# Two dense layers behind an FFT filter on one core: input loads on one queue, eight warm products, another order at the seam and in the last pair

## The chip, the cores and the metric

The kernel runs on one core of a Trainium2 chip. The metric is the device time of one execution in microseconds, taken as the median of several runs. The engines are named as the profile names them: PE (TensorE, matrix products), PEld (its weight loads), DVE (VectorE), ACT (ScalarE), POOL (GpSimd) and SP (SyncE, which here only issues DMAs).

## The reference

```python
X = np.fft.rfft(x, axis=1)                  # x: 2 x 3008 x 256
Y = X * (filt_r + 1j * filt_i)[None, :, :]
x = np.fft.irfft(Y, n=3008, axis=1).reshape(6016, 256)
h = x @ moe_w_in                            # 256 -> 2048
x = np.maximum(0.01 * h, h) @ moe_w_out     # 2048 -> 256
h = x @ moe2_w_in
r = np.maximum(h, 0.0)
out = (r * r) @ moe2_w_out                  # 6016 x 256
```

## The kernel before

**Stage one, the Fourier filter.** 3008 is cut into 64 x 47. The input `X` (128 rows, two batches, 24 steps `m` of 256 channels) comes in 16 pieces, eight for each batch, of 2, 2, 2, 2, 4, 4, 4 and 4 steps (`XG`); a piece of two steps has 256 KB, one of four 512 KB. SP issues 14 of them (L216); pieces 1 and 3 of batch 0 are issued by ACT (`X_BY_ACT`, L506), whose queue also carries the three small matrices `DM`: the first, for the products over n1, ahead of them (L503) and the other two behind them (L507). `over_n1(c, half)` (L872 to L881) is a chunk of four products of 128 columns, one for each step `m`; in single precision each is two instructions in the trace. For the first eight chunks half 0 and half 1 alternate; half 0 waits for a piece of `X` where a step begins one. Ahead of all that PE runs ten products on a cleared tile `WARM` (L869), which DVE clears (L744) and which nothing reads. Then follow, for 32 units, a transposition (`turn`, L895), the products with the tables `TB` (`spectrum`, L906), the filter on DVE and POOL, and the way back (`inverse`, L916), with a trip through memory (`zu`), and at last 24 chunks `sequence(c)` (L934) that give the 6016 tokens in `YT`. ACT and DVE copy these chunks out of PSUM (`y_copy`, lists `Y_ACT` and `Y_DVE`).

**Stages two and three, the dense layers.** The tokens are handled in six pairs of blocks for each layer (five of 2 x 512 tokens and one of 2 x 448), each pair in `KU` = 8 steps over the 2048 hidden values, so there are `SLOTS` = 96 steps `s`. Each 2 x 2 block product is done with seven products instead of eight, by sums of blocks, and each operand is split into a rounded part and a rest (`XH` and `YL`/`XL`, `WIH` and `WIL`, `GH` and `GL`), so that each product is three passes on PE (L973 to L975 upward; L965 to L967 downward). A step has the groups a, b, c and d upward and four down groups, of kinds `UA`, `UB`, `UC`, `UD`, six products each. `UA` and `UC` add to token block 0 (PSUM banks 4 and 5), `UB` and `UD` to block 1 (banks 6 and 7). `down(n)` runs `LAG` = 6 groups behind. The order on every engine is written out by hand, with semaphores for the waits.

**The seam.** Stage two needs pair 0 of the tokens in its forms: sums `x0_t` on DVE, roundings `x_round0(1..6)` on ACT (L561 to L567), rests `x_split0(1..6)` on DVE (L762 to L768). Group a of step 0 waits for rests 1 and 2, group b for 3 and 4, group d for 6. The last four chunks of `sequence` are put between these groups. In each step ACT copies two half-finished products out of PSUM: `snap1` (L621) and `snap2` (L628, into `SN`). Group c, which goes on adding to the same bank, waits for `snap2` (semaphore `s2u_sb`).

```python
            for n in range(4 * SLOTS - LAG, 4 * SLOTS):
                down(n)
```

**The end.** With these two lines PE ends: the last six down groups in the order of their numbers. The result of the last pair leaves in three stores, all issued by SP: block 0 whole, after a copy on ACT (`evacuate(2 * NP - 1, 0)`, L657, both banks in one instruction); row half 0 of block 1, after a copy on DVE (L863), which waits for the first half of the last group; and row half 1 of block 1, after a copy on ACT (L706). SP then waits until all stores have landed.

Of the kernel before, what the change touches and what calls it, by code (L numbers as in the profile page):

```python
# [17 lines left out]
NP = len(PAIR_W)  # L18
KU = FCH // 2
SLOTS = 2 * NP * KU  # L20
XG = (2, 2, 2, 2, 4, 4, 4, 4)
# [7 lines left out]
def fft_mlp_kernel(nc, x, filt, dft, tab, w1i, w1o, w2i, w2o, out):  # L29
# [60 lines left out]
    with ExitStack() as ctx:  # L90
# [75 lines left out]
        Y_ACT = tuple(c for c in range(2 * CH) if c not in Y_DVE)  # L166
        FILL = 2 * CH - 4
        X_START = [sum(XG[:g]) for g in range(len(XG))]
        X_BY_ACT = ((0, 1), (0, 3))
        CHUNKS = 4 * KU  # L170
        W2_IN = (0, 5, 6, 7)
        LATE = 4
# [38 lines left out]
        def _(sp):  # L211
            def load_x(b):
                for g, n in enumerate(XG):
                    m = X_START[g]
                    if (b, g) not in X_BY_ACT:
                        sp.dma_start(X[:, b, m:m + n, :], x[:, b, m:m + n, :]).then_inc(x_in[b][g], 16)  # L216

            def load_filter(f):
                if f >= FSLOTS:
# [3 lines left out]
            def load_table(u):  # L223
                if u in (0, PAIRS - 2):
                    for half in range(2):
                        sp.wait_ge(n1_ps[half], CH // 2 if u == 0 else CH // 2 + 1)
                sp.dma_start(TB[:, u, :, :], tab[:, u, :, :]).then_inc(tb_in[u], 16)
# [19 lines left out]

            load_x(0)
            load_x(1)
            load_table(0)  # L250
            load_table(1)
            load_filter(0)
# [73 lines left out]

            c, w = pair_cols(2 * NP - 1)
            sp.wait_ge(evac[0], 2 * NP)
            sp.dma_start(out[:, :, c:c + w], YT[:, :, c:c + w]).then_inc(out_done, 16)
            sp.wait_ge(last_evac, 1)  # L330
            sp.dma_start(out[:, 0, c + w:c + 2 * w], YT[:, 0, c + w:c + 2 * w]).then_inc(out_done, 16)
            sp.wait_ge(evac[1], 2 * NP)
            sp.dma_start(out[:, 1, c + w:c + 2 * w], YT[:, 1, c + w:c + 2 * w]).then_inc(out_done, 16)
            sp.wait_ge(out_done, 16 * (NP + 2))

        @block.gpsimd
        def _(pool):

            pool.wait_ge(n1_ps[1], CH - LATE + 2)
            nc.gpsimd.memset(XF[32:IM, :, :, :], 0.0).then_inc(xf_pad, 1)  # L340

# [159 lines left out]
        @block.scalar  # L501
        def _(act):
            act.dma_start(DM[:, 0, :], dft[:, 0, :]).then_inc(dft_in, 16)  # L503
            for b, g in X_BY_ACT:
                m, n = X_START[g], XG[g]
                act.dma_start(X[:, b, m:m + n, :], x[:, b, m:m + n, :]).then_inc(x_in[b][g], 16)  # L506
            act.dma_start(DM[:, 1:3, :], dft[:, 1:3, :]).then_inc(dft_rest, 16)  # L507

            for c in range(CH):
                act.wait_ge(n1_ps[0], c + 1)  # L510
# [24 lines left out]
            def wo_round(k):  # L535
                act.wait_ge(wo_raw[k], 16)
                nc.scalar.activation(WOH[:, k, :], WOF[:, wo_slot(k), :], ACT.Copy).then_inc(wo_hi, 1)
# [64 lines left out]
            for c in Y_ACT:  # L602
                if DRAIN <= c < FILL:
                    y_copy(c)
                if c in (4, 6):
                    wi_round(WI_UNITS + (c - 4) // 2)
                if c in (8, 10):
                    wo_round((c - 8) // 2)
                if c == 15:
                    x_round0(1)  # L610
                    x_round0(2)
                if c == 16:
                    x_round0(3)
# [9 lines left out]
            def snap2(s):  # L623

                act.wait_ge(p6_ps, s + 1)
                if s >= 1:
                    act.wait_ge(h_sb[UC], s)
                nc.scalar.activation(SN[:, 0:width(s)], PS[:, XB[s % 2], 0:width(s)], ACT.Copy).then_inc(s2u_sb, 1)  # L628
# [30 lines left out]
            for s in range(SLOTS + 1):  # L659
# [14 lines left out]
                if s == 0:  # L674
                    x_round0(5)
                    x_round0(6)
                    snap2(0)
                if s < SLOTS:
                    g_round(s, UA)
                if k == 1 and p >= 1:  # L680
                    evacuate(p - 1, 1)
                if 1 <= s < SLOTS:
                    snap2(s)
                if s >= 1:
                    g_round(s - 1, UD)
# [15 lines left out]
                    w2_round(s - KU)  # L701

            c, w = pair_cols(2 * NP - 1)
            evacuate(2 * NP - 1, 0)
            act.wait_ge(down_ps, 4 * SLOTS)
            nc.scalar.activation(YT[:, 1, c + w:c + 2 * w], PS[:, 7, 0:w], ACT.Copy).then_inc(evac[1], 1)  # L706

        @block.vector
        def _(dve):
# [28 lines left out]
            def y_copy(c):  # L738

                y, ps = y_cols(c)  # L740
                dve.wait_ge(y_ps, c + 1)
                nc.vector.tensor_copy(y, ps).then_inc(y_done(c)[0], 1)  # L742

            nc.vector.memset(WARM[:, :], 0.0).then_inc(warm_sb, 1)  # L744
            for c in range(CH - 2):
                n1_copy(c)
            filtered(0)
# [35 lines left out]
            nc.vector.tensor_tensor(b12, b22, b12, ALU.subtract).then_inc(x0_t, 1)  # L783
            y_copy(17)
            x_split0(3)
            y_copy(19)
            dve.wait_ge(x0_t, 4)
            x_split0(4)

            def whole_a(s):  # L790

# [67 lines left out]
                    y_copy(23)  # L859

            c, w = pair_cols(2 * NP - 1)
            dve.wait_ge(last_ps, 1)
            nc.vector.tensor_copy(YT[:, 0, c + w:c + 2 * w], PS[:, 6, 0:w]).then_inc(last_evac, 1)  # L863

        @block.tensor
        def _(pe):
            pe.wait_ge(warm_sb, 1)
            for _ in range(10):
                nc.tensor.matmul(PS[:, 0, 0:128], WARM[:, :], WARM[:, :], start=True, stop=True)  # L869
            pe.wait_ge(dft_in, 16)  # L870

# [199 lines left out]
                    sequence(FILL + 3)  # L1071
                down(4 * s - LAG + 3)
            group_d(SLOTS - 1)
            for n in range(4 * SLOTS - LAG, 4 * SLOTS):
                down(n)


def dft_tables():
# [116 lines left out]
```

## Time and profile before

| | us |
|---|---|
| median of 3 runs (lowest, highest) | 1089.81 (1089.57, 1090.07) |
| the profiled execution: its own time | 1089.14 |
| its span | 1087.4 |
| PE busy in it | 1081.5 (99%) |
| DVE, ACT, POOL busy | 771.8, 567.5, 294.9 |

The span runs from the first to the last instruction; 1.7 us of the profiled execution lie outside it. A busy PE is not a PE at its peak: its products overlap, and one that starts late because a clock or an operand was late still counts as busy. So what counts here is when successive products start, and rows of the timeline show that.

### The profile page before, as it was taken

To read this page: it belongs to the slowest core of one execution; us is meant where nothing else is said; L and a number is where in the kernel's file an instruction comes from. 1 tells how busy PE (TensorE), PEld (TensorE's weight loads), DVE (VectorE), ACT (ScalarE), POOL (GpSimd) and SP (SyncE) were. 2 spreads that over 40 slices of the span, in tenths; PEclk is the share of its full clock that TensorE was granted. 3 is DMA by queue.
4 is the path that set the end of the run, shared out by engine and by line. 5 is a ranking of instruction groups with operands and counts; after the bars stand their busy time and mean duration, and the time that the engine had idled before them with its cause. 6 is when DMAs were issued, how large, how long until landed. Compare 5 with 4: busy or idle time off the path is not lost.

```text
span 1087.4 us, 14076 instructions
## 1 busy us (share of the span) xinstructions
PE 1081.5 (99%) x5108; PEld 914.0 (84%) x5108; DVE 771.8 (71%) x1184; ACT 567.5 (52%) x983; POOL 294.9 (27%) x285
## 2 busy tenths in 40 slices
PE   9999999999999999999999999999999999999998
PEld 9888888888888888888899888888888888888997
DVE  2996889777677677676666776776766766766665
ACT  3556655565565565565454554554554554554543
POOL 0789344224234234224220220220220220120000
PEclk9999999999999999999999999999999999999999
DMA  9778400012112212212144200000000000000000
GB/s 319 222 217 274 151 1 1 22 44 59 44 44 54 49 44 54 48 44 55 54 159 158 73 1 1 39 1 1 39 1 1 39 1 1 39 1 1 39 1 34
DMA packets 70053, 66.09 MB, mean 61 GB/s; under 512 B 40800, under 2 KB 55648, under 8 KB 69984
## 3 DMA queue, kind: packets, MB, share of 16 engines
q1 hardware_dynamic: 69408, 64.47, 19.2%
q8 instruction: 41, 0.67, 0.2%
q10 hardware_dynamic: 576, 0.72, 0.2%
q14 instruction: 28, 0.23, 0.1%
HBM read 41.19 MB, written 23.99 MB: 60 GB/s over the span
## 4 chain that ended last, share of the span: by engine, by line
PE 98%; DMA 1%; DVE 1%; ACT 0%; issue 0%; ACTq 0%; DVEq 0%
PE PS L967 16%; PE PS L966 16%; PE PS L965 16%; PE PS L973 14%; PE PS L975 14%; PE PS L974 14%; PE PS L906 3%; PE PS L916 3%; PE PS L879 2%; PE PS L934 1%; PE PS L895 1%; DMA X<-in_x 1%; DVE YL L762 0%; DVE YT L742 0%; DVE XT L780 0%
## 5 line engine op out<-in xcount | busy, mean ns | idle before, releaser
L650 ACT ACTIVATE GH<-GF 128x512 fp32r<-128x512 f32 (+1 forms) x384 | 238.8, 622 | 225.3 <-DVE GF L822 116.3
L828 DVE TENSOR_TENSOR GL<-GF,GH 128x512 fp32r<-128x512 f32 (+1 forms) x384 | 258.6, 680 | 105.2 <-ACT GH L650 99.3
L967 PE MATMUL PS<-GH,WOL 128*128 128x512 f32 (+1 forms) x768 | 295.8, 385 | 0.0
L965 PE MATMUL PS<-GH,WOH 128*128 128x512 f32 (+1 forms) x768 | 295.8, 385 | 0.0
L966 PE MATMUL PS<-GL,WOH 128*128 128x512 f32 (+1 forms) x768 | 295.8, 385 | 0.0
L973 PE MATMUL PS<-XH,WIH 128*128 128x512 f32 (+1 forms) x672 | 259.8, 387 | 0.1
L975 PE MATMUL PS<-XH,WIL 128*128 128x512 f32 (+1 forms) x672 | 258.8, 385 | 0.0
L796 DVE TENSOR_TENSOR GF<-PS,GF 128x512 f32<-128x512 f32 (+1 forms) x96 | 65.3, 680 | 163.8 <-ACT GF L621 163.7
L966 PEld LDWEIGHTS PS<-GL,WOH 128*128 128x128 f32 x768 | 144.2, 188 | 26.9
L965 PEld LDWEIGHTS PS<-GH,WOH 128*128 128x128 f32 x768 | 144.2, 188 | 26.9
L967 PEld LDWEIGHTS PS<-GH,WOL 128*128 128x128 f32 x768 | 144.2, 188 | 26.8
L974 PE MATMUL PS<-YL,WIH 128*128 128x512 f32 (+1 forms) x384 | 147.8, 385 | 0.0
L973 PEld LDWEIGHTS PS<-XH,WIH 128*128 128x128 f32 x672 | 126.2, 188 | 25.7 <-ACT SN L628 1.4
L975 PEld LDWEIGHTS PS<-XH,WIL 128*128 128x128 f32 x672 | 126.1, 188 | 23.5
L621 ACT ACTIVATE GF<-PS 128x512 f32<-128x512 f32 (+1 forms) x96 | 56.5, 588 | 167.0 <-PE PS L967 166.0
L820 DVE SCALAR_TENSOR_TENSOR GF<-GF 128x512 f32<-128x512 f32 (+1 forms) x192 | 142.2, 780 | 1.7
L822 DVE SCALAR_TENSOR_TENSOR GF<-GF 128x512 f32<-128x512 f32 (+1 forms) x192 | 121.6, 673 | 1.7
L974 PE MATMUL PS<-XL,WIH 128*128 128x512 f32 (+1 forms) x288 | 111.0, 385 | 0.0
L421 POOL TENSOR_TENSOR YL<-YT,XH 128x1024 fp32r<-128x1024 f32 (+1 forms) x22 | 52.6, 2390 | 137.9 <-DVE GL L828 137.9
L644 ACT ACTIVATE GF<-PS 128x512 f32<-128x512 f32 (+1 forms) x96 | 56.8, 591 | 57.5 <-PE PS L975 57.5
L974 PEld LDWEIGHTS PS<-YL,WIH 128*128 128x128 f32 x384 | 72.1, 188 | 13.3
L804 DVE TENSOR_TENSOR GF<-PS,GF 128x512 f32<-128x512 f32 (+1 forms) x96 | 64.4, 671 | 0.0
(74 smaller groups left out, 959.1 us busy)
## 6 DMA issues: line engine op xcount, KB each, us to landing
zu<-U SPq DMA_DIRECT2D x32, 192.0 KB, 2.8
V<-zu SPq DMA_DIRECT2D x12, 512.0 KB, 5.4
FL<-in_filt SPq DMA_DIRECT2D x16, 336.0 KB, 4.9
out_y<-YT SPq DMA_DIRECT2D x5, 1024.0 KB, 4.3
X<-in_x SPq DMA_DIRECT2D x8, 512.0 KB, 9.7
wi<-PWH SPq DMA_DIRECT2D x16, 224.0 KB, 2.5
wi<-PWL SPq DMA_DIRECT2D x16, 224.0 KB, 3.1
WIH<-wi SPq DMA_DIRECT2D x8, 448.0 KB, 3.5
```

Of the source, the lines that this page charges most:

```text
L650: nc.scalar.activation(GH[:, g, 0:width(s)], GF[:, g, 0:width(s)], ACT.Copy).then_inc(g_hi[kind], 1)
L796: nc.vector.tensor_tensor(h, PS[:, YB, 0:w], h, ALU.add).then_inc(h_sb[UA], 1)
L804: nc.vector.tensor_tensor(h, PS[:, XB[s % 2], 0:w], h, ALU.add).then_inc(h_sb[UB], 1)
L820: nc.vector.scalar_tensor_tensor(h, h, 0.01, h, ALU.mult, ALU.max).then_inc(g_sb[kind], 1)
L822: nc.vector.scalar_tensor_tensor(h, h, 0.0, h, ALU.max, ALU.mult).then_inc(g_sb[kind], 1)
L828: nc.vector.tensor_tensor(GL[:, g, 0:w], GF[:, g, 0:w], GH[:, g, 0:w].bitcast(f32), ALU.subtract).then_inc(g_lo[kind], 1)
L965: nc.tensor.matmul(acc, wh, xh, start=first, stop=False)
L966: nc.tensor.matmul(acc, wh, xl, start=False, stop=False)
L967: return nc.tensor.matmul(acc, wl, xh, start=False, stop=last)
L973: nc.tensor.matmul(acc, wh, xh, start=first, stop=False, skip_group_check=not first)
L974: nc.tensor.matmul(acc, wh, lo, start=False, stop=False, skip_group_check=not first)
L975: return nc.tensor.matmul(acc, wl, xh, start=False, stop=True, skip_group_check=not first)
```

## The change

- SP issues all 16 pieces of `X` in order, and behind them the second part of `DM`. ACT issues only the first matrix.
- `WARM` is cleared by POOL and no longer by DVE, and PE runs eight products on it and not ten.
- At the seam ACT does `x_round0(1)` ahead of the copy of chunk 15 and not behind it, and in step 1 `snap2(1)` ahead of the rounding `g_round(1, UA)`. DVE does `x_split0(4)` ahead of the copy of chunk 19.
- In the last step the down groups run as UA, UC, UB, UD. Block 0 of the last pair is copied by two engines (ACT bank 4, DVE bank 5) as soon as UC is done and is stored then. The store of row half 1 of block 1 is issued by ACT, on ACT's own queue, right behind ACT's copy.

```diff
--- before.py
+++ after.py
@@ -166,7 +166,6 @@
         Y_ACT = tuple(c for c in range(2 * CH) if c not in Y_DVE)
         FILL = 2 * CH - 4
         X_START = [sum(XG[:g]) for g in range(len(XG))]
-        X_BY_ACT = ((0, 1), (0, 3))
         CHUNKS = 4 * KU
         W2_IN = (0, 5, 6, 7)
         LATE = 4
@@ -212,8 +211,7 @@
             def load_x(b):
                 for g, n in enumerate(XG):
                     m = X_START[g]
-                    if (b, g) not in X_BY_ACT:
-                        sp.dma_start(X[:, b, m:m + n, :], x[:, b, m:m + n, :]).then_inc(x_in[b][g], 16)
+                    sp.dma_start(X[:, b, m:m + n, :], x[:, b, m:m + n, :]).then_inc(x_in[b][g], 16)
 
             def load_filter(f):
                 if f >= FSLOTS:
@@ -247,6 +245,7 @@
 
             load_x(0)
             load_x(1)
+            sp.dma_start(DM[:, 1:3, :], dft[:, 1:3, :]).then_inc(dft_rest, 16)
             load_table(0)
             load_table(1)
             load_filter(0)
@@ -326,16 +325,16 @@
 
             c, w = pair_cols(2 * NP - 1)
             sp.wait_ge(evac[0], 2 * NP)
+            sp.wait_ge(last_evac, 1)
             sp.dma_start(out[:, :, c:c + w], YT[:, :, c:c + w]).then_inc(out_done, 16)
-            sp.wait_ge(last_evac, 1)
+            sp.wait_ge(last_evac, 2)
             sp.dma_start(out[:, 0, c + w:c + 2 * w], YT[:, 0, c + w:c + 2 * w]).then_inc(out_done, 16)
-            sp.wait_ge(evac[1], 2 * NP)
-            sp.dma_start(out[:, 1, c + w:c + 2 * w], YT[:, 1, c + w:c + 2 * w]).then_inc(out_done, 16)
             sp.wait_ge(out_done, 16 * (NP + 2))
 
         @block.gpsimd
         def _(pool):
 
+            nc.gpsimd.memset(WARM[:, :], 0.0).then_inc(warm_sb, 1)
             pool.wait_ge(n1_ps[1], CH - LATE + 2)
             nc.gpsimd.memset(XF[32:IM, :, :, :], 0.0).then_inc(xf_pad, 1)
 
@@ -501,10 +500,6 @@
         @block.scalar
         def _(act):
             act.dma_start(DM[:, 0, :], dft[:, 0, :]).then_inc(dft_in, 16)
-            for b, g in X_BY_ACT:
-                m, n = X_START[g], XG[g]
-                act.dma_start(X[:, b, m:m + n, :], x[:, b, m:m + n, :]).then_inc(x_in[b][g], 16)
-            act.dma_start(DM[:, 1:3, :], dft[:, 1:3, :]).then_inc(dft_rest, 16)
 
             for c in range(CH):
                 act.wait_ge(n1_ps[0], c + 1)
@@ -606,8 +601,9 @@
                     wi_round(WI_UNITS + (c - 4) // 2)
                 if c in (8, 10):
                     wo_round((c - 8) // 2)
+                if c == 14:
+                    x_round0(1)
                 if c == 15:
-                    x_round0(1)
                     x_round0(2)
                 if c == 16:
                     x_round0(3)
@@ -674,12 +670,13 @@
                 if s == 0:
                     x_round0(5)
                     x_round0(6)
-                    snap2(0)
+                if s < 2:
+                    snap2(s)
                 if s < SLOTS:
                     g_round(s, UA)
                 if k == 1 and p >= 1:
                     evacuate(p - 1, 1)
-                if 1 <= s < SLOTS:
+                if 2 <= s < SLOTS:
                     snap2(s)
                 if s >= 1:
                     g_round(s - 1, UD)
@@ -701,9 +698,12 @@
                     w2_round(s - KU)
 
             c, w = pair_cols(2 * NP - 1)
-            evacuate(2 * NP - 1, 0)
+            act.wait_ge(down_ps, 4 * SLOTS - 2)
+            nc.scalar.activation(YT[:, 0, c:c + w], PS[:, 4, 0:w], ACT.Copy).then_inc(evac[0], 1)
             act.wait_ge(down_ps, 4 * SLOTS)
             nc.scalar.activation(YT[:, 1, c + w:c + 2 * w], PS[:, 7, 0:w], ACT.Copy).then_inc(evac[1], 1)
+            act.wait_ge(evac[1], 2 * NP)
+            act.dma_start(out[:, 1, c + w:c + 2 * w], YT[:, 1, c + w:c + 2 * w]).then_inc(out_done, 16)
 
         @block.vector
         def _(dve):
@@ -741,7 +741,6 @@
                 dve.wait_ge(y_ps, c + 1)
                 nc.vector.tensor_copy(y, ps).then_inc(y_done(c)[0], 1)
 
-            nc.vector.memset(WARM[:, :], 0.0).then_inc(warm_sb, 1)
             for c in range(CH - 2):
                 n1_copy(c)
             filtered(0)
@@ -783,9 +782,9 @@
             nc.vector.tensor_tensor(b12, b22, b12, ALU.subtract).then_inc(x0_t, 1)
             y_copy(17)
             x_split0(3)
-            y_copy(19)
             dve.wait_ge(x0_t, 4)
             x_split0(4)
+            y_copy(19)
 
             def whole_a(s):
 
@@ -859,13 +858,15 @@
                     y_copy(23)
 
             c, w = pair_cols(2 * NP - 1)
+            dve.wait_ge(down_ps, 4 * SLOTS - 2)
+            nc.vector.tensor_copy(YT[:, 1, c:c + w], PS[:, 5, 0:w]).then_inc(last_evac, 1)
             dve.wait_ge(last_ps, 1)
             nc.vector.tensor_copy(YT[:, 0, c + w:c + 2 * w], PS[:, 6, 0:w]).then_inc(last_evac, 1)
 
         @block.tensor
         def _(pe):
             pe.wait_ge(warm_sb, 1)
-            for _ in range(10):
+            for _ in range(8):
                 nc.tensor.matmul(PS[:, 0, 0:128], WARM[:, :], WARM[:, :], start=True, stop=True)
             pe.wait_ge(dft_in, 16)
 
@@ -1071,8 +1072,10 @@
                     sequence(FILL + 3)
                 down(4 * s - LAG + 3)
             group_d(SLOTS - 1)
-            for n in range(4 * SLOTS - LAG, 4 * SLOTS):
+            for n in range(4 * SLOTS - LAG, 4 * SLOTS - 4):
                 down(n)
+            for kind in (UA, UC, UB, UD):
+                down(unit(SLOTS - 1, kind))
 
 
 def dft_tables():
```

The input loads on SP, before and then changed. `X<-in_x 128x512` is a piece of two steps, `128x1024` one of four, `in_dft` the small matrices:

```order
0 L210 UNCONDITIONAL_BRANCH
1 L216 DMA X<-in_x 128x512 x2
2 L216 DMA X<-in_x 128x1024 x4
3 L216 DMA X<-in_x 128x512 x4
4 L216 DMA X<-in_x 128x1024 x4
5 L227 DMA TB<-in_tab 112x416 x2
```

```order
0 L209 UNCONDITIONAL_BRANCH
1 L214 DMA X<-in_x 128x512 x4
2 L214 DMA X<-in_x 128x1024 x4
3 L214 DMA X<-in_x 128x512 x4
4 L214 DMA X<-in_x 128x1024 x4
5 L248 DMA DM<-in_dft 128x256
```

Two small pieces came to SP's queue ahead of the four large ones of batch 0, and the rest of `DM` stands between `X` and the tables.

DVE at the seam, before and then changed. `YL<-YT,XH_69` are rests (`x_split0` 2 and 4), `XL_71` is rest 3, `COPY YT<-PS` copies chunks 17 and 19, `GF<-PS,GF` is the first sum of step 0:

```order
107 L783 TENSOR_TENSOR YT<-YT 128x512
108 L742 COPY YT<-PS 128x512 [waits y_ps]
109 L765 TENSOR_TENSOR XL_71<-XT_73,XH_69 128x1024 [waits x0_hi]
110 L742 COPY YT<-PS 128x512 [waits y_ps]
111 L762 TENSOR_TENSOR YL<-YT,XH_69 128x512 [waits x0_hi,x0_t]
112 L796 TENSOR_TENSOR GF<-PS,GF 128x512 [waits s1_sb,p2_ps]
```

```order
106 L782 TENSOR_TENSOR YT<-YT 128x512
107 L742 COPY YT<-PS 128x512 [waits y_ps]
108 L764 TENSOR_TENSOR XL_71<-XT_73,XH_69 128x1024 [waits x0_hi]
109 L761 TENSOR_TENSOR YL<-YT,XH_69 128x512 [waits x0_hi,x0_t]
110 L742 COPY YT<-PS 128x512 [waits y_ps]
111 L795 TENSOR_TENSOR GF<-PS,GF 128x512 [waits s1_sb,p2_ps]
```

The rest and the copy of chunk 19 changed places; nothing else moved there.

ACT in steps 0 and 1, before and then changed. `SN<-PS` is `snap2(1)`, `GH<-GF` are roundings (the letter behind `g_sb` is the kind), `GF<-PS` with `p3_ps` is the copy for kind UD:

```order
104 L650 ACTIVATE GH<-GF 128x512 [waits g_sb_b]
105 L644 ACTIVATE GF<-PS 128x512 [waits p3_ps]
106 L650 ACTIVATE GH<-GF 128x512 [waits g_sb_a]
107 L628 ACTIVATE SN<-PS 128x512 [waits h_sb_c,p6_ps]
108 L650 ACTIVATE GH<-GF 128x512 [waits g_sb_d]
```

```order
103 L646 ACTIVATE GH<-GF 128x512 [waits g_sb_b]
104 L640 ACTIVATE GF<-PS 128x512 [waits p3_ps]
105 L624 ACTIVATE SN<-PS 128x512 [waits h_sb_c,p6_ps]
106 L646 ACTIVATE GH<-GF 128x512 [waits g_sb_a]
107 L646 ACTIVATE GH<-GF 128x512 [waits g_sb_d]
```

`snap2(1)` moved ahead of one rounding.

## Rows read from the trace of the kernel before

**Rows 1.** The page: the chain that ended last, by engine.
```profile
PE 98%; DMA 1%; DVE 1%; ACT 0%; issue 0%; ACTq 0%; DVEq 0%
```

**Rows 2.** Timeline 0 to 30 us: start, duration, engine, line, tiles, count, idle before.
```profile
0.83 0.17 DVE L744 MEMSET WARM<- 128x128 f32 x1 [0.83 <-PEq L1186]
1.05 4.64 PE L869 MATMUL PS<-WARM 128*128 128x128 f32 x20 [1.05 <-DVE WARM L744]
5.48 2.84 PE L879 MATMUL PS<-DM,X 128*128 128x128 f32 x20
8.77 16.85 PE L879 MATMUL PS<-DM,X 128*128 128x128 f32 x148 [0.44 <-DMA X<-in_x]
27.01 1.37 POOL L340 MEMSET XF<- 32x1536 f32 x1 [26.57 <-PE PS L879]
```

**Rows 3.** Windows: stretch, length, busy and starts by engine, PEclk, DMA share, GB/s.
```profile
5.00:6.00 1.00, 1.00 (x7) 1.00 (x6) 0.00 (x0) 0.00 (x0) 0.00 (x0) 1.00 0.99 346
7.00:8.00 1.00, 1.00 (x11) 1.00 (x11) 0.08 (x1) 0.60 (x1) 0.00 (x0) 1.00 0.98 351
10.00:14.00 4.00, 4.00 (x38) 4.00 (x37) 1.40 (x3) 1.31 (x3) 0.00 (x0) 1.00 1.04 409
```

**Rows 4.** Landing: first matrix (ACT 0.7); `X` issued at 0.7, 1.2, 1.7, 8.1.
```profile
DMA to landing us min/median/max: 3.1/3.1/3.1
...
DMA to landing us min/median/max: 2.9/2.9/2.9
...
DMA to landing us min/median/max: 3.7/3.8/3.9
...
DMA to landing us min/median/max: 6.6/6.8/7.1
...
DMA to landing us min/median/max: 13.9/13.9/13.9
```

**Rows 5.** Timeline at the seam, group b of step 0: PE, then DVE.
```profile
119.26 0.40 PE L975 MATMUL PS<-XH,WIL 128*128 128x512 f32 x1
119.75 0.50 PE L973 MATMUL PS<-XH,WIH 128*128 128x512 f32 x1
120.08 0.39 PE L974 MATMUL PS<-YL,WIH 128*128 128x512 f32 x1
...
118.42 0.68 DVE L742 COPY YT<-PS 128x512 f32<-128x512 f32 x1
119.02 0.68 DVE L762 TENSOR_TENSOR YL<-YT,XH 128x512 fp32r<-128x512 f32 x1
```

**Rows 6.** Timeline, group c of step 1: PE, then ACT.
```profile
128.37 0.40 PE L967 MATMUL PS<-GH,WOL 128*128 128x512 f32 x1
128.76 0.50 PE L973 MATMUL PS<-XH,WIH 128*128 128x512 f32 x1
129.10 0.39 PE L974 MATMUL PS<-XL,WIH 128*128 128x512 f32 x1
...
127.59 0.63 ACT L650 ACTIVATE GH<-GF 128x512 fp32r<-128x512 f32 x1 [1.00 <-DVE GF L820]
128.13 0.58 ACT L628 ACTIVATE SN<-PS 128x512 f32<-128x512 f32 x1
```

**Rows 7.** Timeline of the end: PE, DVE, ACT, SP; last row: stores, median to landing.
```profile
1079.26 0.36 PE L965 MATMUL PS<-GH,WOH 128*128 128x448 f32 x1
...
1077.68 1.16 DVE L828 TENSOR_TENSOR GL<-GF,GH 128x448 fp32r<-128x448 f32 x2
...
1083.10 0.54 ACT L706 ACTIVATE YT<-PS 128x448 f32<-128x448 f32 x1 [0.30 <-PE PS L967]
1083.41 0.60 SPq L331 DMA_DIRECT2D out_y<-YT  x1
1084.06 0.67 SPq L333 DMA_DIRECT2D out_y<-YT  x1
...
out_y<-YT SPq DMA_DIRECT2D x2, 224.0 KB, 2.9
```

## The prediction

> **What bounds the kernel now.** I read the chain that ended last first. PE holds 98% of it [rows 1], so time can only be won where PE starts a product later than it could, and behind PE's last product. The timeline shows three such places: the first 9 us, the seam between the filter and the dense layers, and the end. I read each for when products start, since a busy PE hides a late start.
>
> At the start PE runs 20 instructions on the cleared tile from 1.05 us and the first real one starts at 5.48 [rows 2]. They are slow: seven start in the microsecond from 5 us, eleven in the one from 7 us [rows 3], that is one in about 0.213 us and one in 0.112 us. These are 128 columns in single precision at 1.2 and at 2.4 GHz. The clock column says 1.00 in both windows; the spacing shows the clock. The first 20 real instructions start from 5.48 on and the last of them ends at 8.32, so with 0.275 us for that one their 19 steps take 2.57 us; with n slow steps, 0.213n + 0.112(19 - n) = 2.57 gives n = 4.4. So the clock rises at about 6.4 us. The 21st real instruction is due at 8.05 + 0.11 = 8.16 us and starts at 8.77, released by a transfer of `X` [rows 2]. That is piece 3, issued by ACT at 1.7 and landed 7.1 us later; SP's piece 2 and piece 4, issued at 1.2 and 1.6, need 3.7 and 6.6 us [rows 4]. So piece 4 is there at 8.2, before piece 3, which is wanted first.
>
> At the seam a product starts at 119.75 that follows one at 119.26 [rows 5]; 0.23 us is the usual distance for 512 columns (512 at 2.4 GHz are 0.213; 120.08 follows 119.75 by 0.33, one of the late ones). It waits for rest 4 on DVE, which runs from 119.02 to 119.70, behind a copy. The second one starts at 128.76 after 128.37 and waits for `SN`, which ACT writes from 128.13 to 128.71, behind a rounding from 127.59 [rows 6].
>
> At the end PE is done at 1083.1. ACT copies until 1083.64, but SP is still issuing the second store (1083.41 to 1084.01) and issues the third at 1084.06; it lands 2.9 us later, at 1086.95, and the span ends 0.4 us after that [rows 7].
>
> **The change, part by part.**
>
> *Eight warm products.* Four instructions fewer at 0.213 us: the first real one starts 0.85 us earlier, at 4.63, if its data are there. They are: the first matrix lands at 0.7 + 3.1 = 3.9 and piece 0 at 0.7 + 2.9 = 3.7 [rows 4]. PE stays busy without a gap, so I leave the rise at 6.4 us. Then what is won is not 0.85 but four instructions at the fast rate: 4 x 0.112 = 0.45 us. The 21st is due at 7.72.
>
> *One queue.* The value of this is the 0.61 us from 8.16 to 8.77, and 0.10 more because the instruction after the wait starts 0.21 instead of 0.11 us behind: 0.71 us. It is won if piece 3 lands by 7.72. Bounds: in the old order the matrix and pieces 0, 1, 2 and 4 (1.64 MB) were moved by 8.2 us, piece 3 by 8.8. Now piece 3 needs 1.11 MB moved. In proportion, from a start of transfers near 1.9, it lands at 1.9 + 6.3 x 1.11/1.64 = 6.2; the latest is the old 8.7, which would bring nothing of the 0.71 and only what the other parts give. I take 6.2, since landings follow bytes in these rows, and one queue moves 409 GB/s from 10 to 14 us against 346 to 351 for two [rows 3]. Piece 4 is then wanted at 9.06 and was there at 8.2. SP issues two pieces more, some 0.45 us each, while a piece of 256 KB takes 0.7 us to move: hidden by the transfers. The last piece lands at 8.1 + 13.9 = 22.0; its chunk, the 153rd real instruction, starts at 8.77 + 132 x 0.1134 = 23.7 and will at 22.6. So 0.6 us of cover is left, 0.3 more as 128 KB of `DM` now go behind it. Without that cover the start wins 0.5 us less.
>
> *`WARM` on POOL.* DVE clears it in 0.17 us from 0.83 [rows 2]. POOL needs 1.37 us for 1536 columns, so 0.11 us for 128 and a start-up of unknown size: between 0.1 us sooner and 0.2 us later. At the slow clock that counts half. I take zero, as both ends are small.
>
> *Seam.* Rest 4 goes ahead of a copy of 0.60 us of DVE's time: done by 119.10, while PE wants it at 119.49. The wait of 0.26 us and the slow next start (0.33 against 0.23, 119.75 to 120.08) go: 0.37 us. DVE's next sum starts no later, since both still stand before it; chunk 19 is copied 0.6 us later, by 119.7, and PE wants it for its last chunk, which stands behind the group of 119.75, another chunk and group c, over 2 us later. The earlier rounding 1 on ACT lets DVE start its chain of rests sooner, and holds up the copy of chunk 15 by at most its own half microsecond, while chunks of stage one still run on PE and nothing in the rows waits for either: zero. `snap2(1)` is free to run once its product is done. Nine passes of 0.23 us (the other half of group b and six downward) lie between that and the end of the pass of 128.37, so that is near 126.6. It ends at 127.2, and the rounding behind it still starts at 127.59, as it idled 1.00 us for DVE's operand [rows 6]. PE's wait of 0.17 us and the slow next start (0.34 against 0.23) go: 0.28 us. Together 0.65 us; next late is nothing in the 10 us behind, as DVE and ACT are ahead of PE there. The lower bound is 0.3 us, if one of the two only gives way to a wait for another operand.
>
> *End.* PE's work is the same. UC now follows UA and takes the place of UB, which starts at 1079.26; UC before is one group, 1.2 us, later; its last operand, the rest for UC, is ready at 1077.68 + 1.16 = 1078.84 [rows 7]. If that rest were late, it would cost UC what is over 0.42 us. Block 0 is complete 1.2 us earlier, and its store leaves SP free for the next. The last store is issued by ACT right behind its copy, at about 1083.68 and not at 1084.06: 0.38 us. How fast a store lands that ACT issues no row shows. SP's need 2.9 us [rows 7]; the two first loads, issued together, needed 3.1 on ACT and 2.9 on SP [rows 4]. So between 0.18 and 0.4 us; I take 0.38, as it is the same kind of store.
>
> **Sum:** 0.45 + 0.71 + 0.65 + 0.38 = 2.19 us. The profiled execution takes 1089.14, so 1086.95. The median lies 0.67 us higher; I see no reason for that to change and forecast 1089.81 - 2.2 = **1087.6 us**. 0.2% of this kernel, about what a measurement of it can tell from no change, is 2.2 us, so the forecast sits on that border.
>
> **Rivals.**
>
> *The clock rises earlier.* Nothing in one trace says that 6.4 us is fixed. Before, an earlier rise only made PE wait longer for piece 3, so it was worth nothing. Afterwards each microsecond is worth 0.5 us until the pieces are late. One microsecond earlier gives 1087.1; the cover of 0.6 to 0.9 us at the last piece ends the gain at about 1086.8. "TensorE: Matmul & The Clock Gate" of the Trainium skill (part 1, "What you observe") puts the transition at around 4 us after the start, give or take half a microsecond between runs. The row has 5.35 us (1.05 to 6.4). By the page the rise would be at about 5.1, and the time 1087.0.
>
> *The clock rises later, or the store from ACT is slow.* A rise 1 us later costs 0.5 us; a landing of 3.1 us costs 0.2. Either gives 1087.8 to 1088.1.
>
> *One queue carries less than two.* Then piece 3 or the last piece is late and up to 0.7 us of the start is not won: 1088.3. For it speaks that issue on SP is serial; against it the rate of 409 GB/s with one queue. The Trainium skill, "DMA: Bandwidth & Descriptors" ("Issuing engines are not separate DMA queues"), has it that more issuing engines save only issue time; this keeps the chance of this rival low.
>
> *Nothing is won that can be seen*, since the places named are shorter than they look and other waits follow: 1089 and more.
>
> *Slower: a gap behind the eighth warm product.* If the matrix or piece 0 lands after 4.63 us, PE stands still at the slow clock, and if that starts its warming anew the rise comes 5.35 us after the restart. With a restart at 5.5: rise at 10.85, 25 real instructions done by then, where before it was 22 + (10.85 - 8.98)/0.113 = 38. 13 x 0.113 = 1.5 us lost; the seam and the end win 1.03, so 1090.3. It decides from 0.8 us of lateness in a landing on. Against it: 0.7 to 0.9 us of slack, and less traffic beside the first pieces.
>
> **Chances.** The sum as it stands 0.42, earlier rise 0.17, later rise or slow store 0.17, one queue worse 0.11, nothing seen 0.09, slower 0.04. Of the first about half lies beyond 2.2 us, of the second nearly all, of the third and fourth a little: faster 0.44. Slower by over 0.2% is 0.02; the rest, 0.54, is within. The range goes from the early rise with a little to spare, 1086.6, to the cases that win only 0.8 us, 1089.0; about 2 in 10 lie outside.
>
> **What would show it.** 16 instructions on `WARM`; first real one at 4.6; no wait on `X` before 26 us; the long first stretch of L879 ended at about 24.5 instead of 8.77 + 16.85 = 25.6 [rows 2]; no product at the seam more than 0.1 us late; `SN` of step 1 done before 127 (all less the 1.15 us of the start); the last store issued on ACT's queue within 0.1 us of the end of its copy and landed 3 us later; span 1085.2. Wrong would be: a wait on `X` of over 0.2 us, a clock that rises after 7.5 us, a new wait of PE on DVE or ACT between 115 and 130 us, or a last landing that SP's store decides.

## The result, and the profile after

The changed kernel takes 1085.78 us (median of 8 runs, 1085.33 to 1087.02), the kernel before in the same comparison 1089.29 us (8 runs): 3.5 us less, ratio 0.9968 (95% interval 0.9957 to 0.9979). The forecast was 1087.6, its range 1086.6 to 1089.0. The direction was right, and the gain is 1.6 times what the sum gave. A second comparison of the same two kernels (label a_again, below) gave 0.9975 (0.9965 to 0.9985).

| us | before | after |
|---|---|---|
| the profiled execution: its own time | 1089.14 | 1085.68 |
| its span | 1087.4 | 1083.9 |
| first long stretch of products of the filter ends | 25.62 | 24.16 |
| second product of group c, step 1 | 129.10 | 126.85 |
| last product starts | 1082.70 | 1080.46 |
| from there to the end of the span | 4.66 | 3.40 |

Read downward, the two traces are apart by 1.46 us after the start, 2.25 after the seam, 2.24 at the last product and 3.49 at the end. So the start gave 1.46, the seam 0.79, the 950 us between nothing, and the end 1.25 us. For a fair count of the forecast, the kernel before counts too: the forecast started from its first median, 1089.81, and in this comparison it had 1089.29, so 0.5 us of the distance to 1087.6 are not the change.

**The start.** The timeline of PE in the changed kernel, to set beside [rows 2]:

```profile
0.99 3.78 PE L870 MATMUL PS<-WARM 128*128 128x128 f32 x16 [0.99 <-POOL WARM L337]
4.57 19.59 PE L880 MATMUL PS<-DM,X 128*128 128x128 f32 x168
```

The stretch of 168 is in one piece; the wait for `X` behind the twentieth is gone. The windows, to set beside [rows 3], show the clock: seven starts, then twelve.

```profile
5.00:6.00 1.00, 1.00 (x7) 1.00 (x7) 0.00 (x0) 0.00 (x0) 0.00 (x0) 1.00 1.02 393
6.00:7.00 1.00, 1.00 (x12) 1.00 (x11) 0.00 (x0) 0.60 (x1) 0.00 (x0) 1.00 1.02 377
```

In this execution the clock rose from 1.2 to 2.4 GHz near 5.8 us and not 6.4. The landings of the pieces issued at 0.7, 1.2, 1.6, 2.1 and 8.4 us, to set beside [rows 4]:

```profile
DMA to landing us min/median/max: 3.0/3.0/3.0
...
DMA to landing us min/median/max: 3.2/3.2/3.2
...
DMA to landing us min/median/max: 3.6/3.6/3.6
...
DMA to landing us min/median/max: 4.3/4.3/4.3
...
DMA to landing us min/median/max: 12.9/12.9/12.9
```

Piece 3 is there at 2.1 + 4.3 = 6.4 (forecast: 6.2), the last piece at 21.3.

**The seam.** PE and then DVE and ACT, to set beside [rows 5, 6]:

```profile
117.75 0.39 PE L976 MATMUL PS<-XH,WIL 128*128 128x512 f32 x1
117.98 0.39 PE L974 MATMUL PS<-XH,WIH 128*128 128x512 f32 x1
118.21 0.39 PE L975 MATMUL PS<-YL,WIH 128*128 128x512 f32 x1
...
126.40 0.39 PE L968 MATMUL PS<-GH,WOL 128*128 128x512 f32 x1
126.63 0.39 PE L974 MATMUL PS<-XH,WIH 128*128 128x512 f32 x1
126.85 0.39 PE L975 MATMUL PS<-XL,WIH 128*128 128x512 f32 x1
...
116.22 0.69 DVE L761 TENSOR_TENSOR YL<-YT,XH 128x512 fp32r<-128x512 f32 x1
...
124.79 0.60 ACT L624 ACTIVATE SN<-PS 128x512 f32<-128x512 f32 x1
125.41 1.23 ACT L646 ACTIVATE GH<-GF 128x512 fp32r<-128x512 f32 x2
```

All steps are 0.23 us. Rest 4 ends at 116.91, 1.1 us before it is wanted; `SN` ends at 125.39, 1.2 us before.

**The end**, to set beside [rows 7]; the last row is the time from issue to landing of the store that ACT issues.

```profile
1079.12 0.53 SPq L329 DMA_DIRECT2D out_y<-YT  x1
...
1080.86 0.54 ACT L704 ACTIVATE YT<-PS 128x448 f32<-128x448 f32 x1 [1.89 <-PE PS L968]
1080.90 0.34 SPq L331 DMA_DIRECT2D out_y<-YT  x1
1081.43 0.35 ACTq L706 DMA_DIRECT2D out_y<-YT  x1
...
DMA to landing us min/median/max: 2.0/2.0/2.0
```

The issue comes 0.03 us behind the end of the copy, as forecast, but the store lands 2.0 us after its issue, where the sum had 2.9.

### The profile page after: what moved, and what is told of

Its sections match the earlier page's. It is cut to its first block, busy times and chain, and to the rows that moved or that the text cites. A ratio compares the mean times of both kernels' runs of the same rounds, so it can differ in the third digit from the quotient of the medians.

```text
span 1083.9 us, 14070 instructions
## 1 busy us (share of the span) xinstructions
PE 1079.8 (100%) x5104; PEld 914.2 (84%) x5104; DVE 772.2 (71%) x1184; ACT 567.0 (52%) x983; POOL 295.9 (27%) x286
## 3 DMA queue, kind: packets, MB, share of 16 engines
HBM read 41.19 MB, written 23.99 MB: 60 GB/s over the span
## 4 chain that ended last, share of the span: by engine, by line
PE 100%; ACT 0%; issue 0%; POOL 0%; POOLq 0%
PE PS L966 16%; PE PS L968 16%; PE PS L967 16%; PE PS L974 14%; PE PS L976 14%; PE PS L975 14%; PE PS L907 3%; PE PS L917 3%; PE PS L880 2%; PE PS L935 2%; PE PS L896 1%; PE PS L870 0%; ACT YT L704 0%; POOL WARM L337 0%; POOLq L1189 0%
```

## The experiments

First came each part of the change alone, made in the kernel before. The intervals of a comparison are about 0.1% to each side, 1 us, so the medians of the small parts are read together with places in the traces.

**b_act_store: only the last store by ACT.**

```diff
-            sp.wait_ge(evac[1], 2 * NP)
-            sp.dma_start(out[:, 1, c + w:c + 2 * w], ...).then_inc(out_done, 16)
...
+            act.wait_ge(evac[1], 2 * NP)
+            act.dma_start(out[:, 1, c + w:c + 2 * w], ...).then_inc(out_done, 16)
```

> Kernel before, with one edit: the last store is issued by ACT on its own queue behind ACT's copy; block 0 of the last pair still leaves late. Theory A (the stores' bytes queue): before, 896 KB of stores move back to back from 1083.9 to 1086.5 us, so the last landing waits for bytes and not for its issue; issued 0.38 us earlier it still lands within 0.1 us of 1086.9. Change of the time 0.0 to -0.1 us. Theory B (as in the prediction: the issue on SP delays it and the landing takes a fixed 2.9 us): last landing near 1086.6, time -0.38 us. Theory C (a queue of its own makes a store land faster, 2.0 us as in the changed kernel): last landing near 1085.7, time -1.2 us.

Measured 1089.09 us beside 1088.93, ratio 0.9999 (0.9989 to 1.0008). The end of its timeline, and the time to landing of ACT's store:

```profile
1081.91 0.53 SPq L329 DMA_DIRECT2D out_y<-YT  x1
1082.18 0.54 ACT L704 ACTIVATE YT<-PS 128x448 f32<-128x448 f32 x1 [0.29 <-PE PS L967]
1082.50 0.60 SPq L331 DMA_DIRECT2D out_y<-YT  x1
1082.76 0.35 ACTq L706 DMA_DIRECT2D out_y<-YT  x1
...
DMA to landing us min/median/max: 3.3/3.3/3.3
```

It is issued 0.04 us behind the end of the copy, where it was 0.42, and takes 3.3 us to land, where it was 2.9. From the last product to the end of the span there are 4.68 us, before 4.66. Theory A holds; the two others fall. The windows of the kernel before show why (columns as in [rows 3], the last is GB/s):

```profile
1083.50:1084.00 0.50, 0.00 (x0) 0.00 (x0) 0.00 (x0) 0.14 (x1) 0.00 (x0) 1.00 0.00 0
1084.00:1085.00 1.00, 0.00 (x0) 0.00 (x0) 0.00 (x0) 0.00 (x0) 0.00 (x0) 1.00 0.98 366
1085.00:1086.00 1.00, 0.00 (x0) 0.00 (x0) 0.00 (x0) 0.00 (x0) 0.00 (x0) 0.51 1.03 375
1086.00:1086.50 0.50, 0.00 (x0) 0.00 (x0) 0.00 (x0) 0.00 (x0) 0.00 (x0) 0.50 0.94 351
```

From 1084.0 to 1086.5 the DMA engines are full. The three stores have 448 + 224 + 224 KB, 0.92 MB, and that takes 2.5 us at 366 GB/s. The last bytes of the last store stand in a line behind block 0's, and issuing it 0.38 us sooner did not bring them sooner: it landed 4.26 us after the start of the last product, before 4.25.

**b_early_block0: the end as changed, but all stores by SP.** Order of the last groups, copy of block 0 by two engines and its early store.

```diff
-            for n in range(4 * SLOTS - LAG, 4 * SLOTS):
+            for n in range(4 * SLOTS - LAG, 4 * SLOTS - 4):
                 down(n)
+            for kind in (UA, UC, UB, UD):
+                down(unit(SLOTS - 1, kind))
```

> Kernel before, with the end changed except for the issuer: groups UA, UC, UB, UD, block 0 copied by two engines and stored as soon as UC is done; all three stores are issued by SP. Theory A (bytes queue): block 0's bytes have gone when the last store comes; issued by SP right behind the copy, it lands 2.0 to 2.1 us later, near 1085.8; time -1.1 to -1.2 us. Theory B (prediction): the store of block 0 only leaves SP free, 0.38 us at most. Theory C (ACT's queue is what lands fast): landing still 2.9 us after issue, time -0.3 to -0.4 us.

Measured 1087.63 beside 1088.93, ratio 0.9986 (0.9976 to 0.9995): 1.3 us. In its trace:

```profile
1080.53 0.53 SPq L330 DMA_DIRECT2D out_y<-YT  x1
...
1082.31 0.35 SPq L332 DMA_DIRECT2D out_y<-YT  x1
1082.84 0.34 SPq L334 DMA_DIRECT2D out_y<-YT  x1
...
DMA to landing us min/median/max: 2.0/2.0/2.0
```

SP issues the last store and it lands 2.0 us later. From the last product to the end there are 3.42 us; the changed kernel has 3.40. So the whole gain of the end comes from block 0 leaving early (the new order of the groups, the copy by two engines and the early store were run together), and ACT as the issuer adds nothing.

**b_start: the three edits of the start alone.**

> Kernel before, with the three changes of the start alone (one queue, eight warm products, WARM cleared by POOL). Prediction's terms: first transposition (L895 of the old numbering) 1.15 us earlier than 25.45. With the changed kernel's trace (1.46 us earlier, of which 0.29 by a clock that rose at 5.8 instead of 6.4): time -1.1 to -1.6 us, and the transposition follows the rise: 1.15 us earlier if the rise is at 6.4, half a microsecond more for each microsecond that it comes sooner. Rival: the earlier rise comes with the edit (earlier first product), then every run of it shows the rise within 0.1 us of 5.8.

Measured 1087.83 beside 1088.93, ratio 0.9990 (0.9981 to 1.0). The timeline of PE:

```profile
0.99 3.39 PE L864 MATMUL PS<-WARM 128*128 128x128 f32 x16 [0.99 <-POOL WARM L338]
4.22 19.86 PE L874 MATMUL PS<-DM,X 128*128 128x128 f32 x168
```

Sixteen instructions in 3.39 us and not 3.78: here the clock rose at about 3.8 us, while PE was still on `WARM`. The rival (the rise belongs to the edit) falls. But the stretch ends at 24.08, hardly sooner than the changed kernel's 24.16 with its rise at 5.8. At the eleventh product PE was 0.95 us ahead of the changed kernel, as half a microsecond for each microsecond has it. Then it overtook the transfers: two starts were late by 0.30 and 0.20 us, and with the slow steps around them PE had lost 0.88 us by 8.8 us.

**b_seam: the three moves at the seam alone.**

> Kernel before, with the moves at the seam alone (rounding 1 ahead of the copy of chunk 15, snap2(1) ahead of a rounding, rest 4 ahead of the copy of chunk 19). Theory: both late starts on PE (119.75 and 128.76) go, 0.37 + 0.28 us, and small ones beside them: the time falls by 0.65 to 0.85 us. Rival: PE only meets another wait within the next 10 us: under 0.3 us.

Measured 1088.25 beside 1088.93, ratio 0.9997 (0.9987 to 1.0006), which settles nothing by itself. In its trace no product of the dense layers is late at either place. The execution that was profiled had another wait, of PE for a piece of `V` in stage one:

```profile
110.80 1.28 PE L936 MATMUL PS<-DM,V 128*128 128x128 f32 x10
112.62 1.60 PE L936 MATMUL PS<-DM,V 128*128 128x128 f32 x12 [0.55 <-DMA V<-zu]
```

From the first transposition to the product that waits for `SN` of step 9, near 210 us, it took 210.50 - 25.37 = 185.13 us. The kernel before took 210.56 - 25.45 = 185.11, the changed kernel 208.28 - 23.99 = 184.29 and in its second trace (below) 208.85 - 24.51 = 184.34. The product at 112.62 and the one behind it started 0.81 us late in all; without this wait the figure is 184.32. So the seam's 0.8 us stand in three traces, in one of them hidden by a wait of stage one that comes and goes. What the earlier rounding 1 gave by itself was not run.

**b_eight and b_one_queue: the two edits of the start, each alone.**

```diff
-            for _ in range(10):
+            for _ in range(8):
```

> Kernel before with eight warm products instead of ten, loads on two queues as before. Theory: the two edits of the start need each other. PE comes to piece 3 of X sooner and waits longer for it: time 0 to -0.2 us. Prediction's terms taken one by one: -0.45 us. Rival (the gap behind the eighth warm product): the first matrix landed at 3.9 to 4.2 us in all traces and is wanted at 4.6, so no gap; slower only if the first real product starts after 4.9 us.

> Kernel before with all of X and the second part of DM on SP's queue, ten warm products. Theory: piece 3 lands near 6.4 us instead of 7.6 to 8.7, and PE no longer waits for it: -0.71 us where the clock rises late and before waited long, as in the trace of before; over many executions, where the wait was between 0 and 0.7 us, -0.3 to -0.6 us. Rival (one queue carries less): the last piece lands after 22.0 us or some piece is waited for over 0.3 us, and the time stays.

Eight products alone: 1088.83 beside 1088.80, ratio 1.0001 (0.9992 to 1.0010). One queue alone: 1088.03, ratio 0.9993 (0.9984 to 1.0001). The trace of the first is its slowest execution, and shows what can happen with two queues:

```profile
4.63 2.91 PE L879 MATMUL PS<-DM,X 128*128 128x128 f32 x20
9.97 16.29 PE L879 MATMUL PS<-DM,X 128*128 128x128 f32 x143 [2.44 <-DMA X<-in_x]
```

The first real product starts at 4.63 without a gap, but piece 3 of `X` is there only at 9.9. In the five traces in which ACT issued it, it landed between 7.6 and 9.9 us, in the nine in which SP did, between 6.4 and 7.6. By the medians one queue gives 0.8, eight products nothing, and both 1.1. That fits the theory that the products pay only once the piece is not waited for, but 0.3 us is well inside an interval, so it is not shown.

Nor did the kernel before wait for piece 3 every time. In the trace of b_act_store, whose start is the old one, the piece landed at 7.6 us and nothing was late:

```profile
5.48 19.17 PE L879 MATMUL PS<-DM,X 128*128 128x128 f32 x168
```

Its stretch ends at 24.65 us, where the trace before had 25.62.

One queue also has a price that the medians hide. The windows from 3 to 8 us, of the kernel before and of one queue alone:

```profile
3.00:8.00 5.00, 5.00 (x32) 5.00 (x32) 0.08 (x1) 1.50 (x2) 0.00 (x0) 1.00 1.00 362
3.00:8.00 5.00, 5.00 (x36) 5.00 (x36) 0.55 (x1) 0.60 (x1) 0.00 (x0) 1.00 0.99 335
```

Over this stretch the five traces with two queues have 359 to 384 GB/s (mean 372), the nine with one 318 to 369 (mean 349). So one queue moved somewhat less, and the pieces wanted first came sooner all the same, which fits that they stood first. In the trace of one queue alone piece 3 landed at 6.6 us, PE waited for no piece, and the stretch ended at 24.45.

**a_again: the changed kernel once more.**

> The changed kernel once more, so that its parts and the whole are compared with the same kernel before. Sum of the parts run alone, against the kernel before: start -1.1, seam -0.7, end -1.3 us. If they add up, the whole is 3.0 to 3.5 us faster. Its end (last product to the end of the span) 3.4 us. The clock rises at another moment than 5.8 us, as it did in each trace so far (3.8 to 7.0); the first transposition then moves by half of that, unless a piece of X is waited for.

1085.97 beside 1088.80, ratio 0.9975 (0.9965 to 0.9985): 2.8 us, where the parts run alone add up to 1.1 + 0.7 + 1.3 = 3.1 and the first comparison had 3.5. These agree within their intervals. Its start:

```profile
1.00 3.55 PE L870 MATMUL PS<-WARM 128*128 128x128 f32 x16 [1.00 <-POOL WARM L337]
4.39 2.40 PE L880 MATMUL PS<-DM,X 128*128 128x128 f32 x20
7.25 1.60 PE L880 MATMUL PS<-DM,X 128*128 128x128 f32 x12 [0.47 <-DMA X<-in_x]
9.20 15.48 PE L880 MATMUL PS<-DM,X 128*128 128x128 f32 x136 [0.34 <-DMA X<-in_x]
```

The clock rose at about 4.2 us, 1.6 us sooner than in the first trace, and yet the stretch ends at 24.68, 0.5 us later: pieces 3 and 4 landed at 7.2 and 9.1. With an early rise `X` is what binds, and its landings scatter by a microsecond. These two waits are what the prediction named as a sign of being wrong (a wait on `X` of over 0.2 us); the first trace did not have them.

**a_snap: one more move of the same kind.** In the first step of each later pair `snap2` goes ahead of a copy.

```diff
+                if 2 <= s < SLOTS:
+                    snap2(s)
                 if k == 1 and p >= 1:
                     evacuate(p - 1, 1)
-                if 2 <= s < SLOTS:
-                    snap2(s)
```

> Changed kernel with one more move of the same kind: in the first step of each later pair, snap2 is done ahead of the copy of block 1 of the last pair's result (evacuate of block 1) and not behind it. In the trace PE starts late there three times, at 208.3, 290.1 and 371.9 us, by 0.06 and 0.11 us each. Theory: these go, 0.5 us in all against the changed kernel, since the down group that wants the emptied banks comes 0.7 us after group c. Rival: the emptied banks are late instead, at all eleven pairs: 0.1 to 0.3 us each, 1 to 3 us slower.

1085.58 us, ratio 0.9970 (0.9959 to 0.9980), and a second time (a_snap_again) 1085.22, again 0.9970 (0.9959 to 0.9982). In the comparison that also has the changed kernel that is 0.4 us less, inside the interval. The traces show it: in the changed kernel PE starts late at 208.28, 290.09 and 371.90 us,

```profile
208.00 0.39 PE L968 MATMUL PS<-GH,WOL 128*128 128x512 f32 x1
208.28 0.50 PE L974 MATMUL PS<-XH,WIH 128*128 128x512 f32 x1
208.62 0.39 PE L975 MATMUL PS<-XL,WIH 128*128 128x512 f32 x1
```

and in the new one, at the same place, it does not:

```profile
208.57 0.39 PE L968 MATMUL PS<-GH,WOL 128*128 128x512 f32 x1
208.79 0.39 PE L974 MATMUL PS<-XH,WIH 128*128 128x512 f32 x1
209.02 0.39 PE L975 MATMUL PS<-XL,WIH 128*128 128x512 f32 x1
```

The rival (emptied banks come late) did not show: no product behind 130 us is late by over 0.03 us in either trace.

**s_six and s_three: fewer warm products**, on top of that move.

> Changed kernel with the snap2 move of the run before, and six warm products instead of eight. PE has done them at about 3.7 us, and the first matrix lands at 3.9 to 4.2: PE stands still for a few tenths. Theory: a short gap does not hold up the rise; the first real product starts 0.3 to 0.6 us sooner, worth 0.1 to 0.35 us where the clock is what binds and nothing where a piece of X does: time 0 to -0.3 us against the same kernel with eight. Rival (the prediction's slower one: a gap starts the warming anew): the rise comes after 8 us in the trace, and the time is 0.5 to 1.5 us longer.

> The same with three warm products: they end at about 2.4 us, so PE stands still for some 1.5 us before the first real product. Theory (a gap matters for the clock only if it is long): rise between 4 and 9 us as in the other traces, time within 0.4 us of six. Rival (the warming counts from the start of work without a gap): the rise comes 3 to 6 us after the first real product, between 7 and 10 us, and the time is 0.5 to 2 us longer than with eight.

Six: 1085.15, ratio 0.9956 (0.9942 to 0.9969). Three: 1086.59 beside the same 1089.30, ratio 0.9972 (0.9962 to 0.9982), so 1.4 us behind six on the same chip. The start with three:

```profile
0.99 1.65 PE L870 MATMUL PS<-WARM 128*128 128x128 f32 x6 [0.99 <-POOL WARM L337]
3.93 6.23 PE L880 MATMUL PS<-DM,X 128*128 128x128 f32 x34 [1.29 <-DMA DM<-in_dft]
```

Its windows, with 7, 9 and 11 starts:

```profile
7.00:8.00 1.00, 1.00 (x7) 1.00 (x6) 0.25 (x1) 0.00 (x0) 0.00 (x0) 1.00 0.99 352
8.00:9.00 1.00, 1.00 (x9) 1.00 (x9) 0.44 (x1) 0.00 (x0) 0.00 (x0) 1.00 1.03 381
9.00:10.00 1.00, 1.00 (x11) 1.00 (x10) 0.02 (x1) 0.60 (x1) 0.00 (x0) 1.00 1.04 401
```

PE stood still for 1.3 us after the third product, and the clock rose at about 8.5 us, later than in any of the traces in which PE worked on. That is the rival of s_three, in one trace, and the median agrees in direction. Of the 1.4 us between the medians the two traces show 0.70 at the first transposition (25.02 against 24.32), and 0.25 more at a wait for a piece of `V` near 111 us, which has nothing to do with the clock.

**a_snap_again and s_six_again.** To see whether six is better than eight, both once more on one chip.

> The changed kernel with the snap2 move and eight warm products, once more, beside six on the same chip. Expected 3.2 to 3.8 us faster than the kernel before.

> Six warm products once more beside eight. If the 0.9 us by which six stood ahead in the last comparison (against the kernel before, on different chips) was the edit, they stand ahead again by 0.3 us or more; by the theory of the start they are within 0.3 us of each other. Rival: a gap of 0.4 us holds up the rise in some executions; then six is the slower one.

Eight: 1085.22, ratio 0.9970. Six: 1085.33, ratio 0.9968 (0.9956 to 0.9981). The 0.9 us were not the edit; the two cannot be told apart, and with six the short gap of 0.16 and 0.32 us ahead of the first real product did no harm in two traces: the clock rose somewhere between the last warm product, which started at 3.5 us, and the second real one, at 4.3 and 4.5. The best kernel of this study is the changed one with the snap2 move: 3.2 and 3.8 us faster than the kernel before in its two comparisons, 0.4 us beyond the change in the comparison that has both, and 0.5 us by the three late starts in the trace.

**All fourteen traces, part by part.** The medians leave half a microsecond open. The traces do not, outside the start:

| us | without the edit | with it |
|---|---|---|
| first transposition (start) | 24.49 to 25.45 (ten warm products, two queues: 4 traces) | 23.70 to 24.51 (all three edits: 5) |
| from there to the product that waits for `SN` of step 9 (seam) | 185.11 to 185.15 (6) | 184.23 to 184.34 (6) |
| from there to the last product (the later snap2 move) | 872.10 to 872.17 (9) | 871.58 (5) |
| last product to the end of the span (end) | 4.66 to 4.68 (6) | 3.40 to 3.43 (8) |

The second row leaves out b_seam and s_three, which waited for a piece of `V`. Seam and end repeat to a tenth of a microsecond. The start gives 0.85 us between the means, 24.97 and 24.12, and each side scatters by nearly a microsecond.

## Why the prediction was right and wrong

- **What bounds the kernel** was read rightly. PE's late starts and the tail behind its last product were where the time was won: 2.24 us ahead of the last product, 1.25 behind it, nothing else.
- **End, the step that failed.** It stands in the prediction as "The last store is issued by ACT right behind its copy [...]: 0.38 us", with a landing time of 2.9 us taken as a fixed latency, and block 0's early store costed at nothing but an SP that is free. But 0.9 of the 2.9 us were a line: 0.92 MB in three stores, moved in 2.5 us by DMA engines that were full. The same store lands 2.0 us after its issue when block 0's bytes have gone. The term measured 1.25 us (and not 0.38) in the trace and 1.3 us in b_early_block0 alone, and the part that I did price, ACT as issuer, measured nothing (b_act_store). The windows of the old trace had all of it: 366 and 375 GB/s from 1084.0 to 1086.0 us, and 351 in the half microsecond behind. I looked at issue and landing and not at what the engines moved between them. This 0.9 us is the larger part of the 1.3 us by which the gain exceeds the sum in the traces (3.49 against 2.19); 0.3 came at the start and 0.14 at the seam. The time itself lies 1.8 us below the forecast, the other 0.5 by the median of the kernel before: I had seen no reason for its 0.67 us above the profiled execution to change, and over eight runs it was 0.15.
- **Start: 0.45 + 0.71 = 1.16 us, measured 1.46 in the trace and 1.1 by b_start's median.** The sum came out, in part by luck. The 0.71 were read from one execution in which the old start waited for piece 3; in b_act_store's it did not wait at all. b_eight gives nothing and b_one_queue 0.8, which fits that the two terms need each other, but within the noise. The rest of the 1.46 is 0.29 us of a clock that rose 0.58 us sooner in that execution, which the edit did not cause. Piece 3 was forecast for 6.2 us and came at 6.4 (at 6.4 to 7.6 in nine traces). The proportion behind the 6.2 has a slip: 1.64 MB counts piece 3 itself, so it belongs to 8.7 us and not to 8.2, and gives 6.5.
- **Seam: 0.65 us, measured 0.79.** Both late starts went, by 0.37 and 0.28 us as costed. The rest is small late steps, the largest of 0.05 us each at 116.55 and 126.74, which I did not count. No new wait took their place in 10 us or in 950.
- **`WARM` on POOL: taken as zero, between 0.1 sooner and 0.2 later.** POOL starts at 0.74 where DVE started at 0.83 and takes 0.20 us; PE starts 0.06 us sooner.
- **The rival of an earlier clock** was right in that the rise is not fixed: fourteen traces have it between 3.8 and 8.5 us (the two with six warm products somewhere between 3.5 and 4.5). It was wrong in the price of an earlier rise. With a rise at 4.2 (a_again) or 3.8 (b_start) the first stretch ended at 24.68 and 24.08, against 24.16 with a rise at 5.8, because `X` then binds. The bound was set by the last piece's cover; pieces 3 and 4 bound first. In the old kernel an early rise was worth nothing either, for the reason given: with a rise at 4.2 us b_early_block0 waited 0.53 us for piece 3, and its stretch ended at 24.74, where b_act_store with a rise at 5.9 ended at 24.65.
- **The rival "one queue carries less than two".** I held it unlikely by comparing 409 GB/s from 10 to 14 us with 346 to 351 at 5 to 8 us, which are different stretches. In the same stretch, 3 to 8 us, one queue moved 349 GB/s on average and two 372. So it was partly true; in the first trace piece 3 still came in time, and in a_again it did not.
- **The slower rival** (a gap behind the warm products delays the rise) did not decide with eight products: the first matrix had landed by 4.2 us in every trace, and PE had no gap. One trace speaks for its mechanism: three products gave a gap of 1.3 us and a rise at 8.5. Its median lies 1.4 us above that of six products, and the two traces show 0.7 of that at the start.
- **The range** ended at 1086.6, built from the early clock alone. It had no case in which the end gave more than 0.4 us, since I had priced the landing from 2.9 us upward and had no lower end for it. Counted from this comparison's 1089.29 it would have ended at 1086.1, still above 1085.78; counted from a_again's 1088.80 it would have ended at 1085.6, and 1085.97 would have been within.
- What stays open: how the 3.5 and 2.8 us of the two comparisons divide between chips and chance. The parts run alone sum to 3.1 us, between them, and in the table of the traces nearly all the scatter is in the start. What makes the clock rise sooner or later with the same start stays open too.

## What to carry to other kernels

The time from a DMA's issue to its landing is not a latency when others are on their way: before pricing a tail, ask the trace how many bytes the engines move in it and at what rate, and send early whatever can go early, even where nobody waits for it. Two edits that meet at the same wait may have no prices of their own; run each alone and both. A price read from one trace is the price of that execution: look at more than one before a wait goes into the sum. And an instruction order on a hand-scheduled engine is worth a look wherever a copy that no one needs soon stands ahead of one that the bounding engine waits for: here that was two late starts in the change, and three more that one further move took away.

## What the runs showed of the hardware

- PE's clock rose from 1.2 to 2.4 GHz at very different times with the same program start. With first products at 1.0 us and no gap ahead of the rise, eleven traces had it between 3.8 and 7.0 us, that is 2.8 to 6.0 us after the first product, 4.5 in the mean; two with a gap of 0.16 and 0.32 us had it between 3.5 and 4.5. "TensorE: Matmul & The Clock Gate" of the Trainium skill ("What you observe") gives around 4 us, half a microsecond either way; the mean agrees, the scatter here is three times as wide.
- Two queues moved little more than one from 3 to 8 us (359 to 384 against 318 to 369 GB/s), and ACT's queue, which was fed only the pieces wanted early, delivered piece 3 later than the shared queue did (7.6 to 9.9 against 6.4 to 7.6 us). "DMA: Bandwidth & Descriptors" ("Queues, rings and completion order") of the Trainium skill has it that each DMA engine takes turns between the queues it has work for; the rows agree: SP's piece 4 and ACT's piece 3, both issued at 1.7 us, landed at 8.2 and 8.7, the one wanted later ahead of the other.
- At the end of the kernel 366 to 375 GB/s went from SBUF to memory; a store of 224 KB with nothing ahead of it landed 2.0 us after its issue, and SP took 0.34 us to issue such a store, where it took 0.60 and 0.67 with two stores under way.
